# Attention, MoE and MLP on one core: one 768-column ACT copy of the turned probabilities in place of two of 384

## The reference

```
bits of q and k = (x @ proj) > 0          # 6 bits: a bucket of each token
mask   = q bucket == k bucket
scores = where(mask, q @ k.T / 8, -1e9)   # per head, 768 x 768
attn   = softmax(scores); out = attn @ v  # 16 heads
x      = out as 1536 tokens x 512
expert = argmax(x @ w_gate); x = gate * (relu(x @ w1[expert]) @ w2[expert])
h      = x @ w_in; out = elu(h) @ w_out
```

## Time and profile before

| | |
|---|---|
| runs | 958.22, 959.08, 959.59 us; median 959.08 |
| the profiled execution's span, first to last instruction | 958.9 us |
| busy in it | PE 821.8, DVE 467.5, ACT 404.3, POOL 522.0 us |
| attention, 30 to 400 us | PE 289, DVE 268, ACT 245, POOL 250 of 370 us |
| mean clock granted to PE | 0.947 of full |

### The profile page before, as it was taken

The page is one execution under the profiler, slowest core; times in us unless marked ns, Lnnn a source line. Parts: engine busy times, 40 slices in busy tenths (PEclk is TensorE's granted clock), DMA queues, the critical chain, the costliest instruction groups (busy, mean ns, idle before and its releaser), DMA issues.

```text
span 958.9 us, 15201 instructions
## 1 busy us (share of the span) xinstructions
PE 821.8 (86%) x4246; PEld 689.4 (72%) x4247; DVE 467.5 (49%) x809; ACT 404.3 (42%) x803; POOL 522.0 (54%) x700
## 2 busy tenths in 40 slices
PE   4788888888888885099999999992599999999998
PEld 4777776777777774078888777771488788788886
DVE  4777778777777786012222112125643453444333
ACT  3677677676777773022222222120132332334332
POOL 5776767667677662786999999926800000000000
PEclk8899999999999998589999999996799999999999
DMA  3031221111010010554656566633200010001001
GB/s 124 26 102 42 93 73 52 48 34 53 25 46 25 30 53 1 206 176 127 204 186 208 196 197 196 193 93 104 83 11 12 22 45 0 0 0 44 1 1 45
DMA packets 42529, 76.19 MB, mean 79 GB/s; under 512 B 5505, under 2 KB 11649, under 8 KB 42497
## 3 DMA queue, kind: packets, MB, share of 16 engines
q1 hardware_dynamic: 35104, 59.54, 19.5%
q10 hardware_dynamic: 5472, 9.96, 3.2%
q0 software_dynamic: 1920, 6.29, 1.9%
HBM read 59.53 MB, written 16.25 MB: 79 GB/s over the span
## 4 chain that ended last, share of the span: by engine, by line
PE 53%; POOL 17%; issue 15%; DVE 7%; DMA 4%; ACT 3%; POOLq 1%; SPq 0%; ACTq 0%; DVEq 0%
PE ps_s L667 8%; PE ps_s L669 8%; PE ps_s L668 8%; PE ps_t L766 5%; PE ps_t L767 4%; PE ps_t L768 4%; POOL probs L427 4%; POOL w_lo L517 2%; PE ps_o L635 2%; PE ps_p L568 2%; PE ps_t L621 2%; PE ps_o L636 2%; DVE stats L983 2%; PE ps_s L609 2%; PE ps_s L610 2%
## 5 line engine op out<-in xcount | busy, mean ns | idle before, releaser
L983 DVE TENSOR_REDUCE stats<-ps_s 128x1 f32<-128x768 f32 x96 | 91.8, 956 | 53.5 <-PE ps_s L610 53.1
L1003 DVE TENSOR_TENSOR pt_lo<-ps_t,pt_hi 128x384 fp32r<-128x384 f32 x192 | 98.7, 553 | 19.0 <-ACT pt_hi L842 15.8
L851 ACT ACTIVATE probs<-ps_s,stats 128x768 f32<-128x768 f32 x96 | 95.3, 993 | 20.5 <-POOL stats L419 19.7
L427 POOL TENSOR_SCALAR probs<-probs,stats 128x768 f32<-128x768 f32 x96 | 88.0, 917 | 10.1 <-DVE stats L987 1.1
L842 ACT ACTIVATE pt_hi<-ps_t 128x384 fp32r<-128x384 f32 x192 | 84.3, 490 | 19.7 <-PE ps_t L621 17.9
L621 PE MATMUL ps_t<-ident,probs 128*128 128x128 f32 x576 | 84.6, 285 | 6.6 <-POOL probs L427 5.8
L609 PE MATMUL ps_s<-key_hi,query_hi_lo 128*128 128x384 f32 x192 | 70.3, 366 | 21.4 <-DVE key_lo_mask L972 19.4
L517 POOL TENSOR_TENSOR w_lo<-stage,w_hi 128x1024 fp32r<-128x1024 f32 x36 | 86.5, 2403 | 0.0
L517 POOL TENSOR_TENSOR w_lo<-late_stage,w_hi 128x1024 fp32r<-128x1024 f32 x36 | 86.0, 2404 | 0.0
L667 PE MATMUL ps_s<-w_hi,gT_hi 128*128 128x512 f32 x192 | 76.4, 398 | 6.8 <-DVE gT_lo L1181 6.8
L766 PE MATMUL ps_t<-yT_hi,w_hi 128*128 (+1 forms) x192 | 76.4, 398 | 1.9 <-DVE yT_lo L1155 1.4
(11 more groups left out here) (177 smaller groups left out, 1895.9 us busy)
## 6 DMA issues: line engine op xcount, KB each, us to landing
stage<-in_moe_w_dram SPq DMA_DIRECT2D x72, 256.0 KB, 2.9
late_stage<-in_moe_w_dram SPq DMA_DIRECT2D x56, 256.0 KB, 2.9
x_slots<-x_rows SPq DMA_DIRECT2D x19, 256.0 KB, 3.7
xg<-x_slots ACTq DMA_DIRECT2D x19, 256.0 KB, 2.9
y_slots<-y_sb ACTq DMA_DIRECT2D x19, 256.0 KB, 2.7
raw_q<-in_q_dram SPq DMA_DIRECT2D x16, 192.0 KB, 2.4
raw_k<-in_k_dram SPq DMA_DIRECT2D x16, 192.0 KB, 2.5
raw_v<-in_v_dram SPq DMA_DIRECT2D x16, 192.0 KB, 2.4
```

What stands on the lines that cost most here:

```text
L427: g.tensor_scalar(pr, pr, stats[:, 4, (s - 2) % 4:(s - 2) % 4 + 1], 1.0, ALU.mult, ALU.mult).then_inc(normed, 1)
L851: a(probs[:, s % 4].rearrange("p (h c) -> p h c", h=2), ps_s[:, 2 * (s % 2):2 * (s % 2) + 2, 0:HW], ACT.Exp, bias=stats[:, 5, c], scale=st ...
L983: v_.tensor_reduce(stats[:, 0, c], ps_s[:, 2 * (s % 2):2 * (s % 2) + 2, 0:HW], AX.XY, ALU.max).then_inc(max_found, 1)
L1003: v_.tensor_tensor(pt_lo[gb][where], ps_t[:, half, 0:HW].rearrange("p (t c) -> p t c", c=P), pt_hi[gb][where].bitcast(F32), ALU.subtract). ...
```

## The change

ACT waits once, for both halves of `turned`, and copies both banks of `ps_t` with one instruction; its source is two banks of 384 columns, its target the six blocks of 128 columns. It counts `hi_moved` once per unit and not twice. DVE waits for that one count and then does its two subtractions as before.

```diff
@@ -837,10 +837,9 @@
                         gb, uu = (s - 3) // 3 % 2, (s - 3) % 3
                         if uu == 0 and not (first and s < 9):
                             act.wait_ge(weighted, i * 4 + (s - 3) // 3 - 1)
-                        for half in range(2):
-                            act.wait_ge(turned, n * 2 - 6 + half + 1)
-                            a(pt_hi[gb][:, half * HALF:(half + 1) * HALF, uu * P:(uu + 1) * P],
-                              ps_t[:, half, 0:HW].rearrange("p (t c) -> p t c", c=P), ACT.Copy).then_inc(hi_moved, 1)
+                        act.wait_ge(turned, n * 2 - 6 + 2)
+                        a(pt_hi[gb][:, :, uu * P:(uu + 1) * P].rearrange("p (h t) c -> p h t c", h=2),
+                          ps_t[:, :, 0:HW].rearrange("p h (t c) -> p h t c", c=P), ACT.Copy).then_inc(hi_moved, 1)
                     for c in amid:
                         move_chunk(i, *c)
                     if live(i, s, 0, UNITS):
@@ -997,8 +996,8 @@
                         move_chunk(i, *c)
                     if live(i, s, 3, UNITS):
                         gb, uu = (s - 3) // 3 % 2, (s - 3) % 3
+                        dve.wait_ge(hi_moved, n - 3 + 1)
                         for half in range(2):
-                            dve.wait_ge(hi_moved, n * 2 - 6 + half + 1)
                             where = (slice(None), slice(half * HALF, (half + 1) * HALF), slice(uu * P, (uu + 1) * P))
                             v_.tensor_tensor(pt_lo[gb][where], ps_t[:, half, 0:HW].rearrange("p (t c) -> p t c", c=P),
                                              pt_hi[gb][where].bitcast(F32), ALU.subtract).then_inc(lo_moved, 1)
```

## The result

| | before | after |
|---|---|---|
| median of 6 runs | 958.97 us (957.89 to 959.59) | 962.15 us (960.78 to 962.41) |
| ratio, 95% interval | | 1.0032 (1.002 to 1.0043) |

The change makes the kernel 3.2 us slower. The forecast was 6.8 us slower (965.9), with a range of 961.0 to 972.0: the direction holds and the time lies in the range, but the size is off by more than a factor of two.

A forecast was written before the change was run, and what follows sets the result against it. The prediction took attention to be bound by how the engines hand a tile on, with no engine full. Its terms, 2.2 + 2.6 - 0.4 + 0.75 + 1.6 = 6.8 us, on 959.1 gave 965.9 us, range 961.0 to 972.0.

The forecast's parts named there:

- The forecast: Attention: delay through masks, reductions and the end, 6.8 us slower, 965.9 us; chance 0.76.
- Rival B: ACT's joined copy costs as much as the 768-column exponential (0.99 us), giving 971.7 us; chance 0.08.
- `pt_lo` 0.60 us later: DVE's second subtraction starts and ends 0.60 us later, as the copy waits for all six transposes.
- Slot 10, +0.31: Slot 10 of 12 per head pair, pairs 0 to 6: DVE's reduction starts 0.31 us later; 2.2 us in all.
- Slots 1 to 5, +0.44: Pairs 1 to 6: delay through masks 6 and 7 adds 0.44 us per pair; 2.6 us in all.
- Slot 6, nothing: Slot 6 of each head pair: the walk gave it no term in the sum.
- Slot 7, -0.06: Slot 7, six times: the chain goes through ACT's copies, so each saves 0.06 us; -0.4 us in all.
- Pair 7 and the end, 2.35: Last head pair +0.75 us through masks 6 and 7; last units of attention +1.6 us through PE's late transposes.
- The sum, 6.8: Whole of attention: 2.2 + 2.6 - 0.4 + 0.75 + 1.6 = 6.8 us slower.
- Rival C: Clock: shorter PE idle in slot 0 removes half-clock stretches, 1.4 us each; five gone 958.9 us (0.04), six 957.5 (0.04).
- The prediction's own sign of being wrong: Wrong if, among other signs, attention's count of half-clock stretches moves by more than two, which alone is 3 us.
- rival D: ACT bounds attention, so 96 copies at 0.06 us each save 5.8 us, giving 953.3 us; chance 0.02.

The follow-up runs named there:

- e9: Kernel before with eight dummy products on PE in its idle of slot 0 (pairs 1 to 7) and of slot 6 (all pairs): 951.81 us, ratio 0.994.
- e11: Changed kernel with the dummy products on PE in slots 0 and 6: 961.37 us, ratio 1.0043 to the kernel before.
- e2: Changed kernel with eight dummy products on PE in slot 0 of pairs 1 to 7: 961.99 us, ratio 1.0037 to the kernel before.
- e3: Kernel before with the one 768-column copy in slots 1, 2, 6 and 10 alone, two copies in the others: 962.6 us, ratio 1.0043.
- e4: Kernel before with the 768-column copy in the eight slots other than 1, 2, 6 and 10: 957.89 us, ratio 0.9996.
- e7: Kernel before with masks 6, 7 and 8 moved by DVE ahead of its two subtractions: 957.34 us, ratio 0.9999.
- e8: Changed kernel with masks 6, 7 and 8 moved by DVE ahead of its subtractions: 959.49 us, ratio 1.0026 to the kernel before.
- e1: Kernel before with eight dummy products on PE in its idle of slot 0, pairs 1 to 7: 957.08 us, ratio 0.9983.
- e5: Kernel before, still two copies, but ACT's first one waits for both halves of the transposes: 958.75 us, ratio 1.0014.
- e6: Kernel before, still two copies, but DVE's first subtraction waits for both: 958.29 us, ratio 1.0019.
- e10: Kernel before with masks 6, 7 and 8 ahead of the subtractions and dummy products on PE in slots 0 and 6: 951.58 us, ratio 0.9938.

## Why the prediction was wrong, step by step

- **The copy**: 0.81 us forecast, 811 ns measured. Right. Rival B is out.
- **`pt_lo` 0.60 us later**: 0.61. Right.
- **Slot 10, +0.31**: +0.33. Right, with POOL's wait where it was to appear.
- **Slots 1 to 5, +0.44**: 0 to 6 grew by 0.40 to 0.47. Right; PE's idle ahead of mask 6's chunk is 0.39 (forecast 0.4), ahead of mask 7's 1.46 (1.37).
- **Slot 6, nothing**: +0.21. Wrong, and the larger part of what the sum lacks. "The next chunk copy is queued behind the copy" was written down, but the walk followed it only in slot 0, where its reader has time.
- **Slot 7, -0.06**: 0. The next row copy on ACT starts 0.92 us after the pair of copies starts (174.49 to 175.41) and 0.91 after the single one (172.98 to 173.89). It stands 0.21 us behind the end of PE's transposes of `xT` (L591) in both kernels, in each of six pairs, and no copy of `pt_hi` overlaps it. So it goes by PE there and not by the copies; the walk had put their 0.86 us on the chain.
- **Pair 7 and the end, 2.35**: 1.9, from slot 0 of pair 7 to the last `ps_o` in e9 and e11 (47.85 and 49.74 us). About right.
- **The sum, 6.8**: 8.4 without the clock's part (pair 0: 0.3; pairs 1 to 6: 6.3 in e9 against e11, forecast 0.69 x 6 = 4.1; pair 7 and the end 1.9).
- **"The forecast", that the number of half-clock stretches stays**: this is the step that failed, by more than the delay's own error. Rival C named the mechanism, the price of 1.4 us and the place, and had 0.04 and 0.04; the changed kernel had none in pairs 1 to 7, nor had e2, e3 and e11, which share its delay. How many its other executions have isn't recorded, only their mean clock (0.956 to 0.961). The prediction's own sign of being wrong, a count that moves by more than two, came true. I had asked how near the new idle of 1.32 us (1.30 measured) comes to idles with no stretch behind them, and held the one of 1.34 in pair 7 against it, and took the old count as likeliest. The walk weighed one idle by its length, and length is not enough: the rows of the kernel before hold idles of 1.52 and 1.51 us in slot 0 (pairs 3 and 6) with no stretch behind them. Losing a net five in the profile, at 1.4 us each, takes 7.0 from the 8.4; the ends of attention differ by 0.7 us there (372.74 and 373.44).
- **Luck**: the time lies in the range because two errors have opposite signs. The delay was 1.6 us too small, and the clock gave back about 5 that the forecast had at nothing.
- **The base**: the six stretches of the profile were taken for the usual number. By e9 the usual execution loses some 5.6 to 6.1 us to them, about four, and the profiled one was by the estimate 1.6 us above the median. That cost is inside C's price, not in the sum, but it made five or six look like the price of losing all.

The Trainium skill ("Perfetto Trace Analysis", Optimizing Scalar/DVE Operations), weighed in rival D, says that where ACT and DVE aren't saturated but cause bubbles elsewhere, breaking up instructions may let work complete sooner. The runs agree: 8.4 us for undoing a break, with ACT's busy time down by 5 us (404.3 to 399.0).

What stays open: which idle times have a stretch behind them. The table shows PE's idles in us ahead of the scores of slots 0 and 6 and of the chunk behind mask 7, in pairs 1 to 6, and the stretches in slots 0 and 6 of pairs 1 to 7, from one profile of each kernel:

| kernel | pair | idle, slot 0 | mask 7 | idle, slot 6 | stretches in slot 0, slot 6 |
|---|---|---|---|---|---|
| before | 43.4 | 1.51 to 1.54 | 1.27 | 1.27 | 5, 0 |
| e4 | 43.4 | 1.51 to 1.55 | 1.28 | 1.27 | 4, 0 |
| e7 | 43.3 | 1.41 to 1.47 | none | 1.27 | 3, 1 |
| e8 | 43.6 | 1.40 to 1.48 | none | 1.27 | 2, 1 |
| e1 | 43.4 | filled | 1.16 to 1.28 | 1.27 | 0, 3 |
| e5 | 43.7 | 1.26 to 1.31 | 1.18 | 1.27 | 0, 3 |
| e6 | 43.5 | 1.25 to 1.26 | 1.22 | 1.27 | 0, 1 |
| after | 44.4 | 1.25 to 1.31 | 1.46 to 1.47 | 1.27 | 0, 0 |
| e3 | 44.4 | 1.26 to 1.30 | 1.42 to 1.47 | 1.27 | 0, 0 |

One idle of the kernel before, in slot 0 of pair 3, that had none behind it, and the row of slot 6 in e5 that had one:

```profile
147.19 0.44 PE L609 MATMUL ps_s<-key_hi,query_hi_lo 128*128 128x384 f32 x1 [1.52 <-DVE key_lo_mask L972]
...
208.36 0.44 PE L609 MATMUL ps_s<-key_hi,query_hi_lo 128*128 128x384 f32 x1 [1.27 <-DVE key_lo_mask L972]
```

The changed kernel has the idles of e5 in slots 0 and 6 and a longer one ahead of mask 7's chunk, and still no stretch where e5 has three. So a shorter idle of slot 0 goes with stretches leaving slot 0 (e5, e6 and e3 have it too), but it doesn't say why none came in slot 6. The changed kernel and e3 differ from e5 by the length of the pair and by mask 7's idle, and no run takes these two apart. The Trainium skill ("TensorE: Matmul & The Clock Gate", A second HAM failure mode: psum-queue depth-cycling) tells of a kernel whose PE idles briefly but often between groups of matmuls, so that its clock goes back and forth; the traces here agree in kind: six stretches of 3.4 us at half clock in the profile before, with idles of at most 1.54 us ahead of the five in slot 0.

## What to carry to other kernels

Joining two instructions on an engine that isn't full takes away the early handover of the first half; price it by what is queued behind the consumer, and behind the joined instruction itself, in order, at each place of the pattern. Slack hides the first part of the delay and nothing after. Before forecasting less than 1% on a kernel whose PE pauses for a microsecond or more, count the half-clock stretches and learn how their number varies from run to run; one profile is one draw. The length of a pause does not tell whether a stretch follows. Filling such pauses with products nobody reads can be worth more than the edit under study: here 6 us for two of them per pair, 1.5 for one.

## What the hardware showed that was not expected

- A 768-column copy of two banks on ACT is 0.06 us shorter than two of 384, and gives ACT back less than that. In slots 0 and 6, where the next chunk copy is queued directly behind (14 cases in each profile), that one starts 0.71 us after the single copy starts and 0.74 after the two: it overlaps the single copy by 0.11 us and the second of two by 0.13.
- Executions of one kernel ranged over 7 us (953.75 to 960.81), with granted clocks of 0.946 to 0.962 over the whole execution. The clock goes with the time only in part (correlation -0.41 over 35 executions). One part of it is without effect: some profiles (before, e9, e11) have a stretch of 13.7 us at half clock from about 14.8 us on, others (e1, e5, e10) don't. That is 0.007 of the mean clock, and the first chunk of slot 6 in pair 0 starts at 36.9 to 37.0 us in all of them. What else varies, no run isolates. In e9, with the two pauses filled, six executions lie within 2.3 us (950.72 to 952.97).
- With one pause filled the stretches came at another: in e1 in slot 6, behind 1.27 us of idle.
- The part behind attention took 585.2 to 586.2 us from the last `ps_o` to the end in all profiles looked at, so what the kernels differ by arises in attention.
